# State's products of a retention layer as one 256-column product in the score banks, and q's low part on GpSimd alone

## The reference

```python
# first part: a decayed linear attention, B=4, 8 heads, S=768, head dim 64
gamma = 1.0 - 2.0 ** (-5.0 - np.arange(H))
for t in range(S):
    state = gamma * state + einsum('bhd,bhe->bhde', k[:, :, t], v[:, :, t])
    y[:, :, t] = einsum('bhd,bhde->bhe', q[:, :, t], state) / sqrt(D)
x = y.transpose(0, 2, 1, 3).reshape(3072, 512)
# second part: 512 -> 1024, h * softmax(h), layer norm, 1024 -> 512
h = x @ w_in;  u = h * softmax(h);  x = layer_norm(u, g_ln) @ w_out
# third part: 512 -> 2048, h * cos(h), 2048 -> 512
h = x @ w2_in;  out = (h * cos(h)) @ w2_out
```

## Time and profile before

| | |
|---|---|
| median of three runs | 956.09 us (955.62 to 956.10) |
| the profiled execution | 956.15 us, of which its span is 954.4 us |
| TensorE busy | 929.9 us (97%), granted clock 0.989 on average |
| VectorE busy | 732.1 us (77%) |
| ScalarE, GpSimd busy | 562.7 us (59%), 265.2 us (28%) |

### The profile page before, as it was taken

One profiled execution on the slowest core, in us unless ns is written; L12 is line 12 of the kernel. 1 busy time (PEld: TensorE's weight loads), 2 busy tenths in 40 slices (PEclk: granted clock), 3 DMA queues, 4 the chain that ended last, 5 costly groups with the idle time before them and its releaser, 6 DMA issues.

```text
span 954.4 us, 14711 instructions
## 1 busy us (share of the span) xinstructions
PE 929.9 (97%) x4992; PEld 828.8 (87%) x4992; DVE 732.1 (77%) x1054; ACT 562.7 (59%) x923; POOL 265.2 (28%) x260
## 2 busy tenths in 40 slices
PE   3899999999999999999999999999999999999998
PEld 3688888888888888888989999999999999999997
DVE  7989899999999899987756586566776566765564
ACT  5656657657657657646646475545665455656453
POOL 2365576566575676642000000000000000000000
PEclk8799999999999999999999999999999999999999
DMA  7423364533563454538696444734346544354301
GB/s 278 155 67 116 128 227 138 191 139 137 198 214 115 154 198 139 180 105 261 238 328 209 112 128 115 253 111 122 111 126 214 155 114 126 113 186 121 110 12 66
DMA packets 106520, 148.18 MB, mean 155 GB/s; under 512 B 7408, under 2 KB 77040, under 8 KB 106480
## 3 DMA queue, kind: packets, MB, share of 16 engines
q1 hardware_dynamic: 106480, 147.69, 48.1%
HBM read 112.01 MB, written 35.65 MB: 155 GB/s over the span
## 4 chain that ended last, share of the span: by engine, by line
PE 79%; DVE 13%; issue 4%; ACT 2%; DMA 1%; POOL 0%; DVEq 0%; SPq 0%; ACTq 0%; POOLq 0%
PE bank L318 26%; PE bank L321 26%; PE bank L320 26%; DVE p_l L1111 2%; DVE q_l L1095 1%; PE bank L620 1%; DVE work L1161 1%; DVE p_m L1104 1%; DVE nmax L1155 1%; DVE x_l L1135 1%; DVE wo_out L1209 1%; PE bank L655 1%; ACT x_h L788 1%; DVE z_l L1189 1%; DVE s_l L1128 1%
## 5 line engine op out<-in xcount | busy, mean ns | idle before, releaser
L318 PE MATMUL bank<-yc_h,ring 128*128 128x384 f32 x448 | 151.5, 338 | 0.0
L320 PE MATMUL bank<-yc_l,ring 128*128 128x384 f32 x448 | 151.3, 338 | 0.0
L321 PE MATMUL bank<-yc_h,ring 128*128 128x384 f32 x448 | 151.0, 337 | 0.0
L1238 DVE SCALAR_TENSOR_TENSOR gg<-turns,c 128x768 f32<-128x768 int32 x64 | 61.0, 953 | 63.7 <-ACT turns L859 63.7
L1035 POOL TENSOR_TENSOR y_raw<-y_raw,t 128x768 f32<-128x768 f32 x4 | 7.4, 1855 | 361.2 <-DVE yc_l L1220 361.2
L865 ACT ACTIVATE gg<-gg 128x768 f32<-128x768 f32 x64 | 54.1, 846 | 80.2 <-DVE gg L1245 80.1
L859 ACT ACTIVATE turns<-c 128x768 int32<-128x768 f32 x64 | 54.2, 846 | 79.2 <-DVE c L1308 76.7
L318 PEld LDWEIGHTS bank<-yc_h,ring 128*128 128x128 f32 x448 | 84.0, 188 | 8.0 <-issue 0.5
L320 PEld LDWEIGHTS bank<-yc_l,ring 128*128 128x128 f32 x448 | 84.2, 188 | 7.2
L321 PEld LDWEIGHTS bank<-yc_h,ring 128*128 128x128 f32 x448 | 84.0, 188 | 0.0
L318 PE MATMUL bank<-w1i_h,x_h 128*128 128x512 f32 x192 | 79.9, 416 | 3.2 <-DVE x_l L1135 2.5
(11 more groups left out here) (131 smaller groups left out, 2487.6 us busy)
## 6 DMA issues: line engine op xcount, KB each, us to landing
ring<-w_split SPq DMA_DIRECT2D x224, 256.0 KB, 2.8
w_split<-w_out SPq DMA_DIRECT2D x16, 896.0 KB, 4.6
w2o_split<-wo_out SPq DMA_DIRECT2D x16, 512.0 KB, 4.0
w2o<-w2o_split SPq DMA_DIRECT2D x8, 1024.0 KB, 8.7
raw<-kT SPq DMA_DIRECT2D x24, 256.0 KB, 2.6
raw<-qT SPq DMA_DIRECT2D x24, 256.0 KB, 3.0
raw<-kn SPq DMA_DIRECT2D x24, 256.0 KB, 3.8
raw<-vn SPq DMA_DIRECT2D x24, 256.0 KB, 4.7
```

The source lines that it names most:

```text
L318: eng.matmul(dst, ah, bh, start=first and i == 0, stop=False, skip_group_check=read_between)
L320: eng.matmul(dst, ah, bl, start=False, stop=False, skip_group_check=read_between)
L321: m = eng.matmul(dst, al, bh, start=False, stop=last_one and i == n - 1, skip_group_check=read_between)
L1238: dve.scalar_tensor_tensor(gg[:, r, :], turns[:, r, :], -TWO_PI_HI, flat(c_32[:, r, :, :]), ALU.mult, ALU.add)\
```

## The change

The state's products go into the score banks 0 and 1 in place of bank 3. v's high and low part become two planes of one tensor `v_hl`, so that for each pair of heads one matmul of 256 columns gives n's high part times both, side by side, and a second one of 128 columns adds n's low part times v's high part to the first 128 columns. VectorE then adds the two column groups to the state in two steps: first as before (copy, or scale and add), then a `tensor_tensor` with the other 128 columns of each pair, behind a new semaphore `sg_done`. As the banks are shared, DL now waits for the mask products of its own tile (`pm_done`), and SC for the state of the tile before (`st_done`). Apart from that, GpSimd makes both pieces of `q_l`, one after the other, from the third tile on, and then `n_l`; VectorE makes both only in the first two tiles.

```diff
--- before.py
+++ after.py
@@ -102,7 +102,8 @@
         bank = ctx.enter_context(nc.psum_tensor("bank", [128, 8, 512], F32))
         ps_p = bank[:, 0:2, :]
         ps_o = bank[:, 2, :]
-        ps_d = bank[:, 3, :]
+
+        ps_d = bank[:, 0:2, :].rearrange("p g (j a n) -> p (g j) a n", j=2, a=2)
         ps_h = bank[:, 4:6, :]
         ps_t = bank[:, 6, :]
         ps_y = bank[:, 7, :]
@@ -123,7 +124,7 @@
             q_l = sb1("q_l", [128, 2, PAIRS, 2, C], F32R)
             k_h, k_l = sb1("k_h", [128, 2, 512], F32R), sb1("k_l", [128, 2, 512], F32R)
             n_h, n_l = sb1("n_h", [128, 2, 512], F32R), sb1("n_l", [128, 2, 512], F32R)
-            v_h, v_l = sb1("v_h", [128, 2, 512], F32R), sb1("v_l", [128, 2, 512], F32R)
+            v_hl = sb1("v_hl", [128, 2, 2, 512], F32R)
             p_m = sb1("p_m", [128, 2, 512])
             p_h, p_l = sb1("p_h", [128, 2, 512], F32R), sb1("p_l", [128, 2, 512], F32R)
             s_32 = sb1("s_32", [128, 512])
@@ -179,6 +180,7 @@
 
             w2o = sb3("w2o", [128, NF, 2, DM], F32R)
 
+        v_h, v_l = v_hl[:, 0, :, :], v_hl[:, 1, :, :]
         mask = cst[:, MASK0:NCONST].rearrange("p (h t) -> p h t", h=H)
         qsc = cst[:, QSC0:KSC0]
         ksc = cst[:, KSC0:GC0]
@@ -203,6 +205,7 @@
         qk_done = sem("qk_done")
         pm_done, ph_done, pl_done = sem("pm_done"), sem("ph_done"), sem("pl_done")
         d_done = sem("d_done")
+        sg_done = sem("sg_done")
         st_done, sh_done, sl_done = sem("st_done"), sem("sh_done"), sem("sl_done")
         o_done = sem("o_done")
         xh_done, xl_done = sem("xh_done"), sem("xl_done")
@@ -549,6 +552,8 @@
                     wait(pe, k_lo, b, t)
                     for s in q_lo:
                         wait(pe, s, b, t)
+                    if t % TILES > 0:
+                        wait_state(pe, st_done, b, t - 1)
                     for g in range(2):
                         wait(pe, pm_done, b, t - 1, 2, g)
                         for j in range(2):
@@ -562,12 +567,14 @@
 
                     wait(pe, n_lo, b, t)
                     wait(pe, v_lo, b, t)
-                    wait_state(pe, st_done, b, t - 1)
                     for p in range(PAIRS):
+                        if p % 2 == 0:
+                            wait(pe, pm_done, b, t, 2, p // 2)
                         cols = slice(p * 128, (p + 1) * 128)
-                        m = products(pe, ps_d[:, cols], [
-                            (n_h[:, par, cols], n_l[:, par, cols],
-                             v_h[:, par, cols], v_l[:, par, cols])], True, True)
+                        pe.matmul(ps_d[:, p, :, :], n_h[:, par, cols], v_hl[:, :, par, cols],
+                                  start=True, stop=False)
+                        m = pe.matmul(ps_d[:, p, 0, :], n_l[:, par, cols], v_h[:, par, cols],
+                                      start=False, stop=True)
                     m.then_inc(d_done, 1)
                 elif name in ("O0", "O1"):
 
@@ -997,13 +1004,20 @@
                     subtract(v_l[:, par, :], raw[:, par, 3, :], v_h[:, par, :]).then_inc(v_lo, 1)
                 elif name == "PQ" and not by_dve(t, b):
                     wait(pool, q_hi, b, t)
-                    wait(pool, q_lo[0], b, t - 1)
-                    subtract(q_l[0:64, par, :, 0, :], raw[0:64, par, 0, :].rearrange(
-                        "p (c t) -> p c t", c=PAIRS), q_h[0:64, par, :, 0, :])\
-                        .then_inc(q_lo[0], 1)
+
+                    for a in range(2):
+                        wait(pool, q_lo[a], b, t - 1)
+                        if a == 1:
+                            wait(pool, v_lo, b, t)
+                            wait(pool, q_lo[0], b, t)
+                        r = slice(64 * a, 64 * a + 64)
+                        subtract(q_l[r, par, :, a, :], raw[r, par, 0, :].rearrange(
+                            "p (c t) -> p c t", c=PAIRS), q_h[r, par, :, a, :])\
+                            .then_inc(q_lo[a], 1)
                 elif name == "PN" and not by_dve(t, b):
                     wait(pool, n_hi, b, t)
                     wait(pool, n_lo, b, t - 1)
+                    wait(pool, q_lo[1], b, t)
                     subtract(n_l[:, par, :], raw[:, par, 2, :], n_h[:, par, :]).then_inc(n_lo, 1)
                 elif name == "VAR":
 
@@ -1086,15 +1100,13 @@
                     dve.tensor_tensor(n_l[:, par, :], raw[:, par, 2, :],
                                       n_h[:, par, :].bitcast(F32), ALU.subtract)\
                         .then_inc(n_lo, 1)
-                elif name == "PQ":
+                elif name == "PQ" and by_dve(t, b):
                     wait(dve, q_hi, b, t)
-                    if by_dve(t, b):
-                        dve.tensor_tensor(q_l[0:64, par, :, 0, :], raw[0:64, par, 0, :].rearrange(
-                            "p (c t) -> p c t", c=PAIRS), q_h[0:64, par, :, 0, :].bitcast(F32),
-                            ALU.subtract).then_inc(q_lo[0], 1)
-                    dve.tensor_tensor(q_l[64:128, par, :, 1, :], raw[64:128, par, 0, :].rearrange(
-                        "p (c t) -> p c t", c=PAIRS), q_h[64:128, par, :, 1, :].bitcast(F32),
-                        ALU.subtract).then_inc(q_lo[1], 1)
+                    for a in range(2):
+                        r = slice(64 * a, 64 * a + 64)
+                        dve.tensor_tensor(q_l[r, par, :, a, :], raw[r, par, 0, :].rearrange(
+                            "p (c t) -> p c t", c=PAIRS), q_h[r, par, :, a, :].bitcast(F32),
+                            ALU.subtract).then_inc(q_lo[a], 1)
                 elif name == "SC":
                     if isinstance(b, int) and t == 0:
                         dve.wait_ge(ld_mask, 32)
@@ -1114,15 +1126,17 @@
 
                     wait_state(dve, d_done, b, t)
                     wait_state(dve, sl_done, b, t - 1)
+                    s = s_32[:, :].rearrange("p (c n) -> p c n", c=PAIRS)
                     if c == 0:
-                        m = dve.tensor_copy(s_32[:, :], ps_d[:, :])
+                        m = dve.tensor_copy(s, ps_d[:, :, 0, :])
                     else:
                         for p in range(PAIRS):
-                            cols = slice(p * 128, (p + 1) * 128)
                             m = dve.scalar_tensor_tensor(
-                                s_32[:, cols], s_32[:, cols], gam_c[:, p:p + 1], ps_d[:, cols],
+                                s[:, p, :], s[:, p, :], gam_c[:, p:p + 1], ps_d[:, p, 0, :],
                                 ALU.mult, ALU.add)
-                    m.then_inc(st_done, 1)
+                    m.then_inc(sg_done, 1)
+                    wait_state(dve, sg_done, b, t)
+                    dve.tensor_tensor(s, s, ps_d[:, :, 1, :], ALU.add).then_inc(st_done, 1)
                 elif name == "SL" and c < TILES - 1:
                     wait_state(dve, sh_done, b, t)
                     dve.tensor_tensor(s_l[:, c % 2, :], s_32[:, :], s_h[:, c % 2, :].bitcast(F32),
```

## The result

The changed kernel takes 953.74 us in the median of 9 runs (953.22 to 954.6), the one before 956.09 in as many (955.62 to 956.65): ratio 0.9975, 95% interval 0.9965 to 0.9986. It is faster, by 2.4 us (0.25%), where 10.9 were forecast, and lies above the forecast's range, whose high end was 950.2. Its profiled span is 952.0 us, against 954.4 before.

The account below looks back on a forecast made before the run. It took TensorE to bound the iteration, with VectorE having 0.5 us left; gains of 6.8 (DL), 3.0 (x_l waits), 0.4 (last tiles) and 0.7 (start) summed to 10.9 us, from 956.15 to 945.2, range 942.5 to 950.2.

Parts of the forecast that it names:

- Term 1: DL's products on TensorE: block from 1.29 to 0.91 us, 0.38 saved in 18 of 20 DLs, 6.8 us.
- Rival A: The mixed-width DL block is no shorter; terms 2, 3 and 6 stay: 952.0 us, chance 7%.
- Term 2: TensorE's waits for x_l in L1a vanish as VectorE loses q_l: 3.0 us gained.
- Term 3: VectorE's new second add of ST, some 0.70 us: delays no TensorE work, ScalarE's waiting covers its delay; nothing lost.
- Term 4: GpSimd's additional q_l of 1.28 us: q_l and n_l come later but in time, so nothing lost.
- What is late next: O0's wait for p_l, 0.16 us to spare: taken as nothing, bound 14 iterations x 0.38 = 5.3 us.
- Rival B: O0 waits for p_l and DL's saving goes back in up to 14 iterations: 950.5 us, chance 12%.
- Last tiles, 0.4 of gain: A batch's last tile, without DL as cover and p_l already late: freed VectorE helps little, 0.4 us gained.
- Term 6: The start, until 46 us, paced by VectorE: second add costs 0.5, removed q_l gives 1.2, so 0.7 us gained.

Follow-up runs that it names:

- q_only_sh: Kernel before with q_l wholly on GpSimd and ScalarE's rounding of the state behind x_h of O1, 128-column products kept: 953.22 us, ratio 0.9962.
- sh_late: Changed kernel with ScalarE's rounding of the state moved behind x_h of O1: 948.59 us, ratio 0.9924 to the kernel before.
- q_only: Kernel before with q_l on GpSimd as in the change, the three 128-column products kept: 954.42 us, ratio 0.998.
- bank3: Changed kernel with O1's result written to the freed bank 3: 952.48 us, ratio 0.9958 to the kernel before.
- no_add: Changed kernel with the second add of the state left out (output not the reference's): 950.91 us, ratio 0.9935 to the kernel before.
- all_three: Changed kernel with O1's result in bank 3, ScalarE's state rounding behind x_h of O1 and s_l behind the centring: 946.11 us, ratio 0.9899.

## Why the prediction was wrong

In short: the saving at DL and the waits for `x_l` were read rightly, but the forecast took nothing for what is late next. It put nothing on `p_l`, with 0.16 us to spare and a shortened DL, and nothing on the second add. The runs showed both in one loop over VectorE, GpSimd and ScalarE, 17.80 us long, where TensorE's work would allow 17.48.

**Term 1, the products of DL: right in size, wrong in how often it counts.** 0.38 forecast, 0.41 measured. It was counted 18 times; the pairs of `q_only_sh` and `sh_late` show it in the ordinary iterations only, and in the changed kernel as it is 0.09 of it is left there (17.80 against the 17.89 of `q_only`). Rival A is out, the new block took 0.88 us. The gap by columns that the Trainium skill gives for an isolated matmul ("TensorE: Matmul & The Clock Gate", section "Back-to-back issue gap") does not fit this block: by it the block would hardly have changed (an estimate of 0.66 us for 0.67), and it went from 1.29 to 0.88.

**Term 2, the waits for `x_l` in L1a: right as a reading, not as a gain.** They add up to 2.97 us in the trace before, and none is left. But `q_only`, without the new products, gains only 1.6 us from the third score block to the last (370.77 against 372.34), its second tiles are slower and give 0.6 back.

**Term 3, the second add: the step that failed first.** Its size was right (0.69). But "who waits: `x_l` of O0 and U are wanted by L1a" left out O1, which writes the bank that `x_l` of O0 reads and waits for it; in first tiles O1 is 0.5 to 0.6 us late by it, and `bank3` gives 0.6 back. And the cover on ScalarE was read from the kernel before: 0.52 us of waiting for O1. DL's 0.38 brings O1 forward by as much, an estimate of 0.14 left before the add's 0.5 was laid on it. Above all, that wait stands behind `q_h` in ScalarE's queue, so it covers nothing for GpSimd, which waits for `q_h`. `no_add` gives the add's price: 0.32 us in an ordinary iteration, where nothing was forecast.

**Term 4, GpSimd: no one waits for its `q_l` or `n_l`, as said, but `s_l` falls beside `n_l`.** "q's rounding 0.5 later" stood in the text; the second piece and two waits of 0.17 us (the rows of GpSimd above) came on top, and so `n_l` was still running when `s_l` began.

**"What is late next": the decisive step.** It named the instruction (`s_l`, "may lose up to 1 us") and the lack of 0.2 us per iteration, and then took nothing. 0.95 was lost on `s_l`, and `p_l` was late. It also took `p_l`'s 1.17 us as its own length, where `p_l` ended 0.54 us behind GpSimd's `k_l`; so it missed that `s_l`'s delay comes to `p_l` through GpSimd too, and closes the loop. Rival B names what happened at O0, and its bound of 5.3 us was too small, since it counted the return of 0.38 in 14 iterations and no tile that gets slower than before (+1.41 us in the second ones), no O1 that waits in the first ones, and no loss in the start. By the 17.48 us that TensorE needs, what the changed kernel leaves unused in the ordinary iterations alone is 195.74 - 11 x 17.48 = 3.5 us.

**Last tiles, 0.4 of gain: right in sign, and small** (0.73): two of the three gained 1.4 us together, where the wait of 0.93 for `p_l` went, and the first lost 0.7, where one of 0.55 came.

**Term 6, the start: wrong in sign.** 0.7 gain forecast, 0.6 loss measured. VectorE's `w1o_l` in the start, beside GpSimd's second `q_l` and `n_l`:

```profile
40.50 3.11 DVE L1163 SCALAR_TENSOR_TENSOR w1o_l<-w_raw,g_col,w1o_h 128x512 fp32r<-128x512 f32 x2 [0.59 <-ACT w1o_h L808]
```

The same two instructions took 1.42 us before. The removed `q_l` (1.79) came back as 1.7 us on this. But the start differs from kernel to kernel of this study by more than that (the third score block begins at 45.2 to 47.5 us), so its size stays open: no experiment isolates the start.

Most of the forecast sum can be had, as `all_three` shows: with O1's wait for `x_l` of O0 and the add's hold on `q_h` out of the way, and `s_l` moved, the changed kernel gains 9.8 us (955.88 to 946.11), 1.1 short of the forecast 10.9.

## What to carry to other kernels

When an engine is freed and another loaded, list what each then runs side by side: here moving 1.3 us of work to GpSimd took 2.5 us off VectorE and cost it 0.95 us on an instruction that nobody had touched, and reordering one rounding on a third engine gave that back. An instruction that takes longer in the trace than its kind does elsewhere is worth a look at what runs beside it: its end may be another engine's. A slack read from the trace before is spent once: the time that the change itself takes out of the path comes off every slack that is measured against it. And where an engine gets work between two others' steps, follow each of its waiters through PSUM banks too, not only through the data.

## What the runs showed of the hardware

- Some VectorE instructions that start beside one of GpSimd on 512 columns hardly advance until that is over, and nearly always end 0.54 to 0.56 us behind it: `s_l` with two SBUF inputs of 128x512 (1.64 us for 0.69), `p_l` (1.17 for 0.68), the centring of 128x1024 with one (1.64 for 0.75), `w1o_l` (up to 1.76 for 0.75). Those that read PSUM are not slowed: `z_l` takes 0.68 us beside `k_l`, `nmax` 1.21, as without GpSimd.
- It goes the other way too. GpSimd's `n_l`, already running when `s_l` starts, keeps its 1.30 us. Its `k_l`, of the same shape, mostly takes 1.74 us where it starts before VectorE's `wo_out` has ended (156.37, and 156.96 for `wo_out`), and 1.27 to 1.31 where no such instruction is under way.
- In fp32r with new weights each time, four pairs of a 256-column and a 128-column matmul take 0.88 us, 0.22 a pair; two 128-column ones took 0.215 before. The narrow one's successor starts 0.06 us behind it, the wide one's 0.17 to 0.18 in all pairs but the first (0.12).
- A wait of GpSimd on its own last instruction cost 0.17 us, in all 44 cases of each kernel that has it.
